# Row numbers written once, tables in chunks of eight columns, and unused matmuls in the routers' gaps

## The reference

```python
x = attention(q, k, v)                       # (3072, 512)
# layer 1
e_idx = argmax(x @ w_gate);  gate_w = softmax(x @ w_gate)[e_idx]
eom = sigmoid(x @ w_output_gate)
out[mask_e] = gate_w * eom[:, e] * (relu(x[mask_e] @ w1[e]) @ w2[e])
# layer 2, cap = 3072 // 8
for idx in argsort(-logits.flatten()):       # greedy, by falling logit
    tok, e = idx // 8, idx % 8
    if assigned[tok] < 0 and counts[e] < cap: assign
out[mask_e] = relu(x[mask_e] @ w1[e]) @ w2[e]
```

## Time and profile before

| | |
|---|---|
| median of three runs | 1089.0 us |
| profiled execution | 1089.4 us |
| its span (first to last instruction) | 1087.7 us |
| busy share of the span: PE, PEld, DVE, ACT, POOL | 87%, 74%, 66%, 38%, 19% |
| mean clock granted to TensorE | 0.912 of full |
| chain that ended last, by engine | PE 63%, DVE 17%, issue 8%, DVE's sequencer 5%, ACT 2% |

### The profile page before, as it was taken

How to read it: one execution, slowest core, us unless ns; L and a number is a source line. 1 busy time by engine, 2 the same in 40 slices (tenths; PEclk the granted TensorE clock), 3 DMA queues, 4 the chain that set the end, 5 groups by cost and what they waited for, 6 DMA issues and landing times.

```text
span 1087.7 us, 22147 instructions
## 1 busy us (share of the span) xinstructions
PE 944.9 (87%) x6254; PEld 806.8 (74%) x6255; DVE 718.5 (66%) x1889; ACT 411.8 (38%) x885; POOL 202.0 (19%) x249
## 2 busy tenths in 40 slices
PE   7999999986599999999999982444389999999994
PEld 4888888875488888888888862333389999898984
DVE  5888888868775878868887685665536454554521
ACT  3655555645452543525525240000024343343410
POOL 1222222301111111111121111100012123312211
PEclk7999999999699999999999996555579999999998
DMA  9566666434161515425334251000033535444200
GB/s 219 127 144 143 142 142 142 114 114 151 56 235 47 185 48 202 144 96 184 125 116 151 92 186 47 2 2 2 11 126 108 203 122 207 152 167 168 73 30 30
DMA packets 146029, 129.26 MB, mean 119 GB/s; under 512 B 101936, under 2 KB 114224, under 8 KB 145840
## 3 DMA queue, kind: packets, MB, share of 16 engines
q1 hardware_dynamic: 137168, 99.67, 30.5%
q0 software_dynamic: 8800, 28.84, 7.8%
HBM read 107.78 MB, written 20.71 MB: 118 GB/s over the span
## 4 chain that ended last, share of the span: by engine, by line
PE 63%; DVE 17%; issue 8%; DVEq 5%; ACT 2%; ACTq 1%; DMA 0%; POOL 0%; POOLq 0%
PE ps_o L1220 10%; PE ps_s L1197 9%; PE ps_o L1593 8%; PE ps_s L1577 6%; PE ps_pT L1577 6%; DVE product L1420 5%; PE ps_o L493 4%; PE ps_s L1593 4%; PE ps_pT L474 3%; PE ps_t L1754 3%; PE ps_s L461 2%; DVE arena_p L668 2%; PE ps_pT L1208 1%; DVEq L675 1%; DVEq L1423 1%
## 5 line engine op out<-in xcount | busy, mean ns | idle before, releaser
L1220 PE MATMUL ps_o<-w_split_parts,hs 128*128 x696 | 168.3, 398 | 9.1 <-ACT hs L1297 9.1
L1197 PE MATMUL ps_s<-w_split_parts,xs 128*128 x696 | 168.0, 397 | 1.4 <-ACT xs L1289 0.9
L1220 PEld LDWEIGHTS ps_o<-w_split_parts,hs 128*128 128x128 f32 x696 | 130.1, 190 | 36.7 <-issue 10.1
L1420 DVE SCALAR_TENSOR_TENSOR product<-y_sb,wg_all 128x512 bf16<-128x512 f32 x232 | 150.9, 688 | 6.9 <-ACT y_sb L1315 1.9
L1197 PEld LDWEIGHTS ps_s<-w_split_parts,xs 128*128 128x128 f32 x696 | 130.4, 191 | 27.8 <-issue 2.0
L777 ACT ACTIVATE arena_p<-arena_p,min_s 128x256 f32<-128x256 f32 (+1 forms) x192 | 91.7, 484 | 12.1 <-DVE min_s L657 11.3
L1593 PE MATMUL ps_o<-w_split_parts,hs 128*128 128x512 f32 x384 | 94.6, 398 | 0.0
L1411 DVE TENSOR_TENSOR w_split_parts<-raw,w_split_parts 128x1024 f32 (+1 forms) x68 | 78.7, 1220 | 5.8 <-ACT w_split_parts L1308 4.6
L1593 PEld LDWEIGHTS ps_o<-w_split_parts,hs 128*128 128x128 f32 x384 | 70.2, 188 | 16.5 <-ACT hs L1627 2.9
L1673 DVE TENSOR_TENSOR w_split_parts<-raw,w_split_parts 128x1024 fp32r<-128x1024 f32 x56 | 68.7, 1226 | 20.2 <-ACT w_split_parts L1635 20.1
L1315 ACT ACTIVATE y_sb<-ps_o,gates 128x512 f32<-128x512 f32 x29 | 20.0, 688 | 162.7 <-DVE logits L1425 118.6
(11 more groups left out here) (294 smaller groups left out, 1723.3 us busy)
## 6 DMA issues: line engine op xcount, KB each, us to landing
raw<-in_moe_w SPq DMA_DIRECT2D x32, 2048.0 KB, 9.0
y_rows<-y_sb POOLq DMA_DIRECT2D x31, 256.0 KB
kn<-in_k SPq DMA_DIRECT2D x32, 192.0 KB, 3.5
qn<-in_q SPq DMA_DIRECT2D x32, 192.0 KB, 3.6
vn<-in_v SPq DMA_DIRECT2D x32, 192.0 KB, 2.8
x_rows<-arena_x SPq DMA_DIRECT2D x96, 64.0 KB, 1.6
va<-in_v SPq DMA_DIRECT2D x32, 120.0 KB, 2.6
wg_rows<-in_moe_w_gate SPq DMA_DIRECT2D x1, 2048.0 KB, 7.6
```

Source lines behind the costliest of these rows:

```text
L1197: last = nc.tensor.matmul(ps_s[:, f, :], xs[:, a, c * P:(c + 1) * P], weights(par, w, cols), start=(n == 0), stop=(n == len(passes) - 1))
L1220: last = nc.tensor.matmul(ps_o[:, 0, :], hs[:, a, c * P:(c + 1) * P], weights(par, 2 + w, slice(c * DM, (c + 1) * DM)), start=(n == 0), st ...
L1420: nc.vector.scalar_tensor_tensor(product[:, e % 2, :], y_sb[:], 1.0, wg_all[:, e, :], ALU.mult, ALU.mult, accum_out=log_now[:, e:e + 1])
```

## The change

`row_no` becomes a tensor of its own, 128 x 8 a partition, written once by GpSimd among its constants, and serves for rows and blocks alike: the block is now compared as a block number instead of as a multiple of 128, and every chunk has at most eight columns, so that the same eight columns serve for each. `hot` is made per chunk. The semaphore `numbered` and both calls of `number` go. `step_f` moves into `xg` and `blk_f` into `wide`, which frees the room. TensorE gets matmuls of 512 columns whose result nobody reads (`keep_busy`): 18 after the first table, 2 after each count, 1 after the first three moves of a phase, 8 after each tally, 16 after the second table. `product` is set to zero once, so that they read defined data.

```diff
+PART = 8
+        row_no = sb("row_no", [P, P, PART], bf16)
-        step_f = sb("step_f", [WAYS, 4, WAYS])
+        step_f = xg[0:WAYS, 0:4 * WAYS].rearrange("p (j w) -> p j w", j=4)
-        blk_f = sb("blk_f", [1, BLK1, E])
+        blk_f = wide[0:1]
         def chunks(cols):
-            half = cols // 4 * 2 if cols % 4 == 0 else (cols + 1) // 2
-            return [range(0, half), range(half, cols)]
+            return [range(a, min(a + PART, cols)) for a in range(0, cols, PART)]
+        def keep_busy(count):
+            for _ in range(count):
+                nc.tensor.matmul(ps_o[:, 1, :], product[:, 0, 0:P], product[:, 0, :], start=True, stop=True)
...
-            done(nc.vector.tensor_copy(pos_i[:, 0:cols], pos[:, 0:cols]))
+            nc.vector.tensor_copy(pos_i[:, 0:cols], pos[:, 0:cols])
+            done(nc.vector.tensor_scalar(t2[:, 0:cols], pos[:, 0:cols], 1.0 / P, None, ALU.mult))
             done(nc.vector.tensor_scalar(key_i[:, 0:cols], pos_i[:, 0:cols], P - 1, None, ALU.bitwise_and))
             nc.vector.tensor_copy(pos_r[:, 0:cols], key_i[:, 0:cols])
-            done(nc.vector.tensor_tensor(pos_b[:, 0:cols], pos[:, 0:cols], key_i[:, 0:cols], ALU.subtract))
+            done(nc.vector.scalar_tensor_tensor(pos_b[:, 0:cols], key_i[:, 0:cols], -1.0 / P, t2[:, 0:cols], ALU.mult, ALU.add))
-            dve.wait_ge(numbered, numbers)
-            some = even(range(0, cols))
-            wide_hot = [P, blocks, some.stop]
-            nc.vector.tensor_tensor(hot[:, 0:blocks, some], block_no[:, 0:blocks, some],
-                                    pos_b[:, some].unsqueeze(1).to_broadcast(wide_hot), ALU.is_equal)
+            def of_row_no(rows, here):
+                return row_no[:, 0:rows, 0:here.stop - here.start]
             for part in chunks(cols):
                 here = even(part)
-                done(nc.vector.tensor_tensor(row_hot[:, :, here], row_no[:, :, here],
+                nc.vector.tensor_tensor(hot[:, 0:blocks, here], of_row_no(blocks, here),
+                                        pos_b[:, here].unsqueeze(1).to_broadcast([P, blocks, here.stop - here.start]), ALU.is_equal)
+                done(nc.vector.tensor_tensor(row_hot[:, :, here], of_row_no(P, here),
                                              pos_r[:, here].unsqueeze(1).to_broadcast([P, P, here.stop - here.start]), ALU.is_equal))
                 dve_vals(part, sets, blocks, parts).then_inc(row_hots, 1)
...
                 last.then_inc(counted, 1)                       # count_above
+                keep_busy(2)
...
                                  skip_group_check=True).then_inc(moved, 1)   # move
+                if j < FAST - 1:
+                    keep_busy(1)
...
                 ... rise, start=True, stop=True).then_inc(tallied, 1)       # tally, end of phase
+                keep_busy(8)
...
-            pe_table(pe, ps_t[:], WIDE_CHUNKS, BLK1, 4, BLK2)
+            pe_table(pe, ps_t[:], HOT_CHUNKS, BLK1, 4, BLK2)
+            keep_busy(16)
...
+            g.memset(product[:], 0.0)
+            g.iota(row_no[:], [[1, P], [0, PART]], base=0, **exact)
...
-            def number():
-                g.iota(block_no[:], [[P, BLK1], [0, COLS]], base=0, **exact)
-                g.iota(row_no[:], [[1, P], [0, COLS]], base=0, **exact).then_inc(numbered, 1)
-            pool.wait_ge(lx_turned, TILES)
             pool.wait_ge(x_stored, 16 * PAIRS * QT)
-            number()
             pool_experts(pool)
-            number()
             pool_experts2(pool)
...
             pe_table(pe, ps_t[:], 0, TILES, 2, BLK1)            # first router
+            keep_busy(18)
             pe_experts(pe)
```

More of the change, by code:

```diff
@@ L181, in program @@
          gate, key_a, key_b, code_taken, e_a, e_b, e_c, room, room_open, count, short_, tally_, rise_, most_, step_now_,
-         row_hot_, hot_, vals_, row_no_, block_no_) = carve(
+         row_hot_, hot_, vals_) = carve(
             arena_t, [BLK1 * 2 * E, NE, NE, NE, NE, NE, NE // 2, NE // 2, BLK1 * WAYS // 2] + [COLS] * 13
-            + [E] * 6 + [E, E, E, 1, WAYS // 2 + 1, P * COLS // 2, BLK1 * COLS // 2, NV // 2, P * COLS // 2, BLK1 * COLS // 2])
+            + [E] * 6 + [E, E, E, 1, WAYS // 2 + 1, P * COLS // 2, BLK1 * COLS // 2, NV // 2])
         hi_, lo_ = hi, lo
@@ L201, in program @@
         step_now = step_now_[0:WAYS].bitcast(bf16)[:, 0:WAYS]
-        row_hot, row_no = grid(row_hot_.bitcast(bf16), P, COLS), grid(row_no_.bitcast(bf16), P, COLS)
-        hot, block_no = grid(hot_.bitcast(bf16), BLK1, COLS), grid(block_no_.bitcast(bf16), BLK1, COLS)
+        row_hot, hot = grid(row_hot_.bitcast(bf16), P, COLS), grid(hot_.bitcast(bf16), BLK1, COLS)
         vals_all = vals_.bitcast(bf16)
@@ L283, in program @@
         tabled = sem("tabled")
-        numbered = sem("numbered")
         tables = sem("tables")
@@ L1009, in dve_vals, with dve_positions @@
                                            parts[:, :, here].unsqueeze(2).to_broadcast(shape), ALU.mult)
-        def dve_positions(dve, prods, cols, blocks, exact, parts, numbers, first=True):
+        def dve_positions(dve, prods, cols, blocks, exact, parts, first=True):
             def done(_):
@@ L1082, in dve_routing1 @@
             nc.vector.tensor_tensor(lw[:, 0:C, :], logits, col_b(m, C), ALU.subtract).then_inc(r_s, 1)
-            dve_positions(dve, 1, C, BLK1, False, token_parts, 1)
+            dve_positions(dve, 1, C, BLK1, False, token_parts)
             ids, at = ps_t[:, 0:BLK1], ps_t[:, BLK1:2 * BLK1]
@@ L1093, in dve_routing1 @@
             nc.vector.tensor_copy(slot_parts[:, 3, 0:BLK1], at)
-            done(nc.vector.tensor_tensor(blk_f[:], iota_b[0:1].unsqueeze(2).to_broadcast([1, BLK1, E]),
+            done(nc.vector.tensor_tensor(blk_f, iota_b[0:1].unsqueeze(2).to_broadcast([1, BLK1, E]),
                                          e_c[0:1].unsqueeze(1).to_broadcast([1, BLK1, E]), ALU.is_ge))
-            done(nc.vector.tensor_reduce(blk_e[:], blk_f[:], AX, ALU.add))
+            done(nc.vector.tensor_reduce(blk_e[:], blk_f, AX, ALU.add))
             done(nc.vector.tensor_scalar(blk_e[:], blk_e[:], float(E - 1), None, ALU.min))
@@ L1737, in program @@
         PHASES = E - 1
-        WIDE_CHUNKS = len(chunks(TILES)) * 2
+        HOT_CHUNKS = len(chunks(TILES)) * 2
         def pe_routing2(pe):
@@ L1795, in pe_routing2 @@
                 pe_ranks(pe, 3, BLK1)
-                pe_table(pe, ps_t[:], WIDE_CHUNKS + len(chunks(BLK1)), BLK1, 4, BLK2)
+                pe_table(pe, ps_t[:], HOT_CHUNKS + len(chunks(BLK1)), BLK1, 4, BLK2)
         def dve_routing2(dve):
@@ L1973, in slow_phase @@
                 done(nc.vector.tensor_tensor(code_all, code_all, code_taken, ALU.add))
-            dve_positions(dve, 2, C, BLK2, True, slot_parts, 2)
+            dve_positions(dve, 2, C, BLK2, True, slot_parts)
             dve.wait_ge(tabled, 3)
@@ L1990, in dve_routing2 @@
                 nc.vector.tensor_tensor(cm(one_hot_bf, C), exp_b(code_e, C), col_b(code_all, C), ALU.is_equal).then_inc(r_v, 1)
-                dve_positions(dve, 3, C, BLK2, True, slot_parts, 2, False)
+                dve_positions(dve, 3, C, BLK2, True, slot_parts, False)
                 dve.wait_ge(tabled, 4)
```

2 lines of the change are left out of this document (1 added, 1 removed).

## The result

The changed kernel takes 1091.26 us (median of 9 runs, 1089.39 to 1093.78); the kernel before, on the same chip, 1088.21 (9 runs, 1085.82 to 1091.14). The ratio is 1.003, with a 95% interval of 1.0016 to 1.0044: slower by about 3 us, where 12 us faster had been forecast; 1091.3 lies above the upper end of the range, 1090. The profiled execution took 1091.26 us, span 1089.5.

A forecast was written before the change was run, and what follows sets the result against it. It took the routers' 152 us to be bound by short VectorE operations and matmuls alternating, TensorE mostly at its lower clock. Terms -3.4 + 0.2 - 1.5 - 2.2 - 2.7 - 2.4 = -12.0 took 1089.4 to 1077.4 us; range 1071 to 1090.

The forecast's parts named there:

- Row numbers: Ahead of the second router: without GpSimd's second iota, VectorE's 2x2 `diag` is no longer held; 3.4 us gained.
- Attention: Writing `row_no` and zeroing `product` on GpSimd beside attention might hold a VectorE operation; 0.2 us lost.
- Chunks of eight: Router tables: less VectorE work ahead of the second table's first matmul, 1.5 us gained; first table net 0.
- 18 behind the first router: Unused matmuls in 5.75 idle us bring the clock back for the first expert tile and transposes; 2.2 us gained.
- The search: Second router's 28 steps: first phase loses 1.15 us at the lower clock, six gain 0.64 each; 2.7 gained.
- 16 behind the second router: Unused matmuls in 6.15 idle us raise the clock for the second experts' first tile and transposes; 2.4 us gained.
- A: Clock comes and goes in the search, four phases low and three high: search +2.7, total 1083 us; chance 0.20.
- B: Clock stays low in the whole search, only dense runs behind the routers raise it: search +8.0, 1088 us; chance 0.15.
- D: Fillers fit but bring nothing, small matmuls bound by issue, clock lost before first full tiles: 1084.5 us; chance 0.07.
- Rival C: Fillers never raise the clock and each is paid at 0.43 us: +6.2, 1095 us; chance 0.08.

The follow-up runs named there:

- no_fill: The changed kernel without any of its unused matmuls (18, 2, 1, 8 and 16): 1083.61 us, ratio 0.9943 to the kernel before.
- entry_only: The changed kernel with unused matmuls only behind the two tables (18 and 16), none in the search: 1081.36 us, ratio 0.9918 to the kernel before.
- gather_first: entry_only, with SyncE requesting the second expert's second weights' first half only after the third row gather landed: 1080.97 us, ratio 0.992 to the kernel before.
- search_only: The changed kernel with unused matmuls only in the search (2, 1 and 8), without the 18 and 16: 1094.58 us, ratio 1.0043 to the kernel before.

## Why the prediction was wrong

The sum had six terms; this is what each became in the changed kernel.

- **Row numbers, -3.4: right.** The operation takes 0.22 us, as forecast; the nine other kernels without the iota have 374.6 to 375.2 in that column against 378.5. In the changed kernel itself only 3.0 is seen, since the last tile ahead of it took 8.59 us (7.70 before): its clock was 0.50 for the first 6 us of it, before for 4.
- **Attention, +0.2:** +0.1 in the trace, within what this column varies by between runs (268.3 to 269.4).
- **Chunks of eight, -1.5:** 1.2 in the second table (`no_fill`). The part that hung on the upper clock, 0.3, never came.
- **18 behind the first router, -2.2:** the mechanism was right, with the clock back as forecast and the tile at 5.77; the 17 that the trace holds took 5.01 us. Against `no_fill` they bring 1.9 here and 2.9 in `entry_only`, but `no_fill` is itself 1.0 longer here than before (first tile 8.30 us, not 7.70: the clock came back later), so against before it is 0.9 and 1.9, and 3.0 in `gather_first`. I had written that the weight queue does not eat it, since the blocks move forward together. It was looked at in the wrong place: the gather that comes behind the request for weights took 7.4 to 9.0 us instead of 6.3, and ahead of it GpSimd's tiny copy took 1.18 instead of 0.18, beside a VectorE operation with two inputs. In the changed kernel TensorE stood still 1.9 us around the late gather; in `entry_only` it did not wait for it, and what was lost there was the clock, 0.51 from 297.3 to 300.7. `gather_first` shows that the order of the two requests sets the gather's length (3.3 us).
- **The search, -2.7: the step that failed**, and by itself more than the whole miss. It came out at +7.6, of which 0.5 stands in `no_fill` as well, and +0.65 in the ranks behind it. Three parts of it were wrong. (1) "The search starts at the lower clock, so I give the first phase to it": the clock did rise behind the eights, once a phase, and fell again within a count or two, once within three. The six phases at the upper level were six short stretches. The earlier trace rows had shown just this, a clock falling under small matmuls, and I put it in a rival at 0.20. (2) The gain at the upper level was taken as 0.64 a phase, 0.4 of it for four steps, and these bring 0.02 each: for 28 steps at the upper level that is 0.6 us, an estimate from the two periods. The other 0.25, the tally's, no trace shows, since no tally ran at that level. (3) The price at the lower level, 1.15 a phase, was 1.5 (`search_only`, 10.4 in seven), because a count's fillers push the move by 0.24 and not 0.15, and because the eight behind the last tally stand ahead of the ranks.
- **16 behind the second router, -2.4:** the two columns behind `rows_i` are 1.6 shorter than before, but 0.6 of it comes without them (`no_fill`), so theirs is 1.0. They raised the clock, and behind 1.46 idle us it was lost again in the first tile (5.97, where 4.2 were possible). The prediction had named that gap and taken the gain all the same.

Of the rivals, A (the clock comes and goes) was right on the clock and priced the search at +2.7. B had the cost nearly right, +8.0 against 8.2, but for a clock that stays low: at 0.55 on average (`search_only`) the same fillers cost 10.4. D had the reason right for the counts, which do not follow the clock, and was wrong that the fillers fit. With 8.2 in place of -2.7 the sum of the forecast gives -12.0 + 10.9 = -1.1, and with the 1.3 that are missing from the 18's term, 0.8 in the 16's, 0.3 in the table's and 0.4 in the first term, it comes to +1.7, what the two traces show (+1.8). Rival C, the only one priced on the slower side, is refuted: the fillers behind the tables do raise the clock.

The underlying error is that of a gain worked out for a resource (clock) without asking whether the operations there are bound by it. The earlier trace rows could have told: 23 more matmuls of 8 columns take 1.01 - 0.35 us, 29 ns each, where 8 columns at the pace of the earlier trace rows (0.43 us for 512 at the lower clock) would need 7. Those wide ones halve with the clock (0.43 to 0.21); the narrow ones stay at 32 ns each at either level, and what sets that pace no run here shows.

## What to carry to other kernels

In this kernel unused matmuls paid only ahead of wide matmuls, whose pace follows TensorE's clock; ahead of counts of eight columns they brought nothing that shows, and cost time wherever they outlasted the gap. Put them behind the last small operation of a stage and ahead of a dense one, and size each lot by the gap at the lower clock (here that was the level at which they mostly ran): two at 0.43 us in a gap of 0.66 were the dearest edit here, 7.5 us over 28 steps. When a stage is brought forward, look at which DMA is then asked for first on another queue. And where the clock's return differs from one execution to the next, read a gain of 1 to 3 us from several runs, not from one pair of traces.

## What was not expected of the hardware

- A 2x2 operation of VectorE held for 4.01 us by GpSimd's iota comes back with the iota alone, without any semaphore (3.3 us in the time, 3.6 in the trace).
- The granted clock fell to 0.50 while TensorE was busy for 1.7 to 2.0 of every 2 us with small matmuls and fillers, and rose at the end of 3.6 us of fillers alone.
- The clock fell at the first tile of the second experts in three kernels and not in a fourth, though in all four 16 fillers had raised it and TensorE had stood idle for the same 1.46 us just before (first tile 5.85 to 5.99 us against 4.40). What decides this stays open.
- A gather of 128 rows took 3.3 us when 2 MB of weights were asked for behind it, and 6.3, 7.4 and 9.0 us when they were asked for about 2.6, 0.9 and 0.9 us ahead of it.
